# Attention in front of two feed-forward layers: the output product of a pair moved from step 3 to step 1, and its PV products spread over three steps instead of two

## The reference

```python
scores = q @ k.T / sqrt(64)                  # per batch (4) and head (8): 576 x 576
scores = where(block_i >= block_j, scores, -1e9)   # blocks of 64 rows and columns
attn = exp(scores - max(scores))
attn = attn / (sum(attn) + 1e-9)
x = attn @ v                                 # (4, 8, 576, 64) -> (2304, 512)
x = (sigmoid(x @ w_gate) * (x @ w_val)) @ w_out      # d_ff 1536
out = top-1 mixture of 8 experts (x, w_gate, w1, w2) # 2304 x 512
```

## Time and profile before

| | |
|---|---|
| median of 3 runs | 1006.93 us |
| lowest, highest | 1004.75, 1008.24 us |
| profiled execution, its own time | 1004.57 us |
| its span in the profile | 1002.8 us |
| PE busy over the span | 914.2 us (91%) |
| DVE, ACT, POOL busy | 338.6, 298.5, 253.0 us |
| attention | from 0 to about 230.7 us of the span |
| stretch 100 to 200 us: PE, DVE, ACT busy | 78.39, 65.16, 47.87 us of 100 |
| PE on the chain that ended last | 70% of the span |

### The profile page before, as it was taken

One profiled execution on the slowest core, in us unless ns is written; L12 is line 12 of the kernel. 1 busy time (PEld: TensorE's weight loads), 2 busy tenths in 40 slices (PEclk: granted clock), 3 DMA queues, 4 the chain that ended last, 5 costly groups with the idle time before them and its releaser, 6 DMA issues.

```text
span 1002.8 us, 15746 instructions
## 1 busy us (share of the span) xinstructions
PE 914.2 (91%) x5370; PEld 758.2 (76%) x5371; DVE 338.6 (34%) x635; ACT 298.5 (30%) x654; POOL 253.0 (25%) x249
## 2 busy tenths in 40 slices
PE   7788777769999999999999999999388998999995
PEld 3444444438999999999999999999367887888884
DVE  5665666662121110120120120111744445235421
ACT  4443444542222122112111211211254344125310
POOL 4033333311121111111111111111253445225521
PEclk9999999999999999999999999999689999999998
DMA  4443444432220010010010000000374547115310
GB/s 130 136 150 107 137 140 147 134 117 89 74 63 32 1 32 32 1 32 13 21 32 1 32 1 1 32 1 1 118 267 160 184 155 258 42 42 209 120 42 30
DMA packets 45536, 83.08 MB, mean 83 GB/s; under 512 B 6831, under 2 KB 19119, under 8 KB 45488
## 3 DMA queue, kind: packets, MB, share of 16 engines
q1 hardware_dynamic: 39728, 67.21, 20.8%
q0 software_dynamic: 3360, 10.49, 3.2%
q10 hardware_dynamic: 2400, 4.72, 1.2%
HBM read 68.17 MB, written 14.75 MB: 83 GB/s over the span
## 4 chain that ended last, share of the span: by engine, by line
PE 70%; POOL 2%; issue 2%; DMA 1%; DVE 1%; ACT 0%; POOLq 0%; ACTq 0%; SPq 0%; DVEq 0%
PE bank L1162 21%; PE bank L1163 21%; PE bank L1164 21%; PE bank L1299 2%; PE bank L1221 1%; DMA stage<-in_we 1%; POOL ew1l L368 1%; PE bank L1212 1%; PE bank L1273 1%; POOL ew2l L368 0%; PE bank L1129 0%; PE bank L1264 0%; POOL yg L598 0%; POOL out L615 0%; POOL ag L587 0%
## 5 line engine op out<-in xcount | busy, mean ns | idle before, releaser
L1162 PE MATMUL bank<-xh,w1h 128*128 128x384 f32 x576 | 196.1, 340 | 0.0
L1164 PE MATMUL bank<-xh,w1l 128*128 128x384 f32 x576 | 193.3, 336 | 0.0
L1163 PE MATMUL bank<-xl,w1h 128*128 128x384 f32 x576 | 193.2, 335 | 0.0
L573 POOL TENSOR_TENSOR hl<-hraw,hh 128x384 fp32r<-128x384 f32 x72 | 77.1, 1071 | 406.5 <-ACT hh L701 406.5
L889 DVE TENSOR_TENSOR hraw<-sig,bank 128x384 f32<-128x384 f32 x72 | 39.9, 554 | 349.2 <-ACT sig L730 349.2
L730 ACT ACTIVATE sig<-bank 128x384 f32<-128x384 f32 x72 | 35.4, 492 | 262.6 <-PE bank L1164 262.6
L672 ACT ACTIVATE prob<-bank,nmax 128x576 f32<-128x576 f32 (+2 forms) x144 | 76.1, 529 | 118.1 <-DVE nmax L842 112.9
L1162 PEld LDWEIGHTS bank<-xh,w1h 128*128 128x128 f32 x576 | 108.3, 188 | 1.8
L1163 PEld LDWEIGHTS bank<-xl,w1h 128*128 128x128 f32 x576 | 108.3, 188 | 1.7
L1164 PEld LDWEIGHTS bank<-xh,w1l 128*128 128x128 f32 x576 | 108.1, 188 | 0.0
L1090 PE MATMUL bank<-kt,qt 64*64 64x64 f32 (+7 forms) x640 | 71.7, 441 | 15.6 <-ACT prob L672 10.3
(11 more groups left out here) (147 smaller groups left out, 1306.8 us busy)
## 6 DMA issues: line engine op xcount, KB each, us to landing
stage<-in_we SPq DMA_DIRECT2D x56, 512.0 KB, 4.4
w1raw<-in_w SPq DMA_DIRECT2D x8, 768.0 KB, 5.5
kt<-in_kT SPq DMA_DIRECT2D x16, 288.0 KB, 3.7
qt<-in_qT SPq DMA_DIRECT2D x16, 288.0 KB, 4.2
rwide<-rinv_scratch SPq DMA_DIRECT2D x32, 144.0 KB, 3.1
xt_scratch<-xo SPq DMA_DIRECT2D x16, 288.0 KB, 2.1
xraw<-xt_scratch SPq DMA_DIRECT2D x6, 768.0 KB, 4.7
y_scratch<-yrow ACTq DMA_DIRECT2D x6, 768.0 KB, 3.6
```

Source lines behind the costliest of these rows:

```text
L573: pool.tensor_tensor(hl[:, f % 2, :], hraw[:, f % 2, :], hh[:, f % 2, :].bitcast(F32), ALU.subtract).then_inc(h_low, 1)
L1162: pe.matmul(out_, wh, ah, start=first, stop=False, skip_group_check=True)
L1163: pe.matmul(out_, wh, al, start=False, stop=False, skip_group_check=True)
L1164: return pe.matmul(out_, wl, ah, start=False, stop=last, skip_group_check=True)
```

## The change

It makes four edits:

1. The output product of pair g - 2 moves on DVE from step 3 to step 1.
2. PV's key tiles 3 and 4 move on PE from step 6 to step 8; tiles 1 and 2 stay in step 6, tile 0 in step 4.
3. SP stores `xo` before the reciprocals instead of after them, since the output product now comes ahead of the reciprocals.
4. After the last pair, DVE does the copy of unit 8, the output product of pair 14, the reciprocals of pair 15 and then the subtraction for `xl`.

```diff
-        PV_STEP = {4: [0], 6: [1, 2, 3, 4]}
-        RSUM_STEP, O_STEP = 2, 3
+        PV_STEP = {4: [0], 6: [1, 2], 8: [3, 4]}
+        RSUM_STEP, O_STEP = 2, 1
...
                 if not early:
-                    rinv_store(g - 2, p % 2)
                     if p == 3:
                         o_store(b, 0)
                     elif not isinstance(b, int):
                         o_store(b - 1, p + 1)
+                    rinv_store(g - 2, p % 2)
                     rwide_load(g - 2, p % 2)
...
             xload(0, PPB)
+            o_store(BATCH - 1, PPB - 3)
             rinv_store(NPAIR - 2, 0)
-            o_store(BATCH - 1, PPB - 3)
             rwide_load(NPAIR - 2, 0)
+            o_store(BATCH - 1, PPB - 2)
             rinv_store(NPAIR - 1, 1)
-            o_store(BATCH - 1, PPB - 2)
             rwide_load(NPAIR - 1, 1)
...
-            recips(NPAIR - 1, 1)
...
-            for i in range(NB - LAG, NB):
-                after_unit(NPAIR - 1, 1, i)
+            after_unit(NPAIR - 1, 1, NB - LAG)
+            after_unit(NPAIR - 1, 1, NB - LAG + 1)
+            o_out(NPAIR - 2, 0)
+            recips(NPAIR - 1, 1)
+            after_unit(NPAIR - 1, 1, NB - 1)
             xlow(0, 0)
-            o_out(NPAIR - 2, 0)
             o_out(NPAIR - 1, 1)
```

## The result

| | before | changed |
|---|---|---|
| median | 1006.99 us | 990.64 us |
| lowest to highest | 1004.75 to 1008.24 | 989.87 to 993.07 (4 runs) |
| profiled execution, its span | 1004.57, 1002.8 | 989.87, 988.2 |
| first feed-forward product | 230.74 | 213.01 |
| first w_out product | 243.33 | 226.23 |

The changed kernel is faster, by 16.4 us: ratio 0.9845, interval [0.9822, 0.9868]. The forecast was 982. The forecast for the first feed-forward product was a gain of 24.4; there the profiled execution is 17.7 ahead, and at its end 14.7.

What follows compares the result with a forecast made beforehand. No engine is full in attention; PE waits each pair for DVE's output product. Gains 14.6 (pairs) + 7.0 (end) + 2.8 (clock) - 0.2 = 24.2 us off 1004.57 give 980.4, stated as 982; range 970 to 992.

Steps and rivals of the forecast that it cites:

- the circle: Pair loop over DVE, ACT and PE: 13.50 us period, PE waiting for the output product before PV; 12.4 us forecast.
- half the gain: Rival for the whole kernel: splitting PV gives nothing and clock falls stay, gain 14.6 us, time 990; chance 0.18.
- The clock: PV steps behind two of fourteen waits for xo: both clock falls vanish with shorter waits, 2.8 us gained.
- The end of attention: Last pair to first feed-forward product: earlier transposes, product and PV at full clock gain 7.0 us; 5.5 without the clock.
- The output product to step 1: DVE, each pair: product ahead of the third reduction lets PV start 1.12 us earlier; 0.77 without earlier scores 1 and 2.
- PV in three steps: PE, each pair: moving key tiles 3 and 4 ends PE's 0.37 us idle and DVE's 0.35, total PE work unchanged.
- With the gap gone I take full clock: Last PV on PE: without the 4.76 us idle it runs at full clock, 3.1 us instead of 4.57, 1.5 gained.
- I take back 0.2: First w_out products: last output product ends only 3.2 to 4.4 us earlier, so 0.2 us of the gain is lost.
- The cover: Slack that keeps new waits away: 3.3 us at w_out, 2.5 us at K's scaling; rwide's load 4.3 us early.
- `rwide` late: Rival in step 1: the load of rwide lands too late and holds DVE and PE every pair, 1037 us; chance 0.05.

Runs made afterwards that it cites:

- e1: Changed kernel with PV back in two steps, so only the output product, SP's order and the end are changed: 994.07 us, ratio 0.9885.
- e2: Kernel before with PV in three steps and nothing else: 1005.49 us, ratio 0.9987.
- e7: Changed kernel as it is, timed and profiled a second time: 989.98 us, ratio 0.9823.
- e10: Changed kernel with the slice of w1 issued right behind the little store of the reciprocals instead of 4.4 us ahead: 989.17 us, ratio 0.9834.
- e3: Kernel before with only the new order after the last pair, on DVE and SP: 1002.68 us, ratio 0.9962.
- e4: Changed kernel with SP's old order, the little store of the reciprocals ahead of the big store of xo: 990.52 us, ratio 0.9832.
- e5: Changed kernel with the output product moved earlier again, to step 8 of the pair before: 991.15 us, ratio 0.9839.
- e6: e5 with PV in two steps, tiles 1 to 4 in step 6: 979.07 us, ratio 0.9726.
- e8: e6 with SP's old order, the little store of the reciprocals ahead of the big store of xo: 976.62 us, ratio 0.9696.
- e9: e6 with the slice of w1 issued right behind the little store instead of 4.9 us ahead of it: 977.05 us, ratio 0.9718.

## Why the prediction was right or wrong

The direction, the circle and the range were right; the time, 990.64 against 982, came out near the range's upper end, outside the 976 to 987 that the forecast's own sum had: the range held since it took in the rivals. That is the figure of the rival "half the gain", but only half for its reason: the clock falls stay, while the split does give something. Up to the PV step at 200.94 (212.84 before) 11.9 us were won, where the forecast says 13 x 1.12 + 1.12 + 2.8 = 18.5; from there to the first feed-forward product 5.8, where it says 24.4 - 18.5 = 5.9. Of the missing 6.7 the steps account for 6.5:

| step of the forecast | forecast | measured | missing |
|---|---|---|---|
| first reduction to PV | 4.65 | 4.73 | 14 x 0.08 = 1.1 |
| PV to the next first reduction | 7.73 | 7.87 | 13 x 0.14 = 1.8 |
| "The clock" | 2.8 | 0 (two falls before, two after) | 2.8 |
| intervals into pairs 4, 8 and 12 | as others | 12.76, 12.94, 12.86 | 0.7 |
| "The end of attention", from that PV step on | 5.9 | 5.8 | 0.1 |

The two intervals ahead of the loop are 12.46, together 0.3 us shorter than reckoned, and each fall costs 1.5 instead of 1.4, so the last digit of the sum means little.

- **"The output product to step 1": right in mechanism, too large.** e1 measured 0.61 for the part that the forecast put at 0.77. Three hand-offs make up the rest. The third reduction came 3.08 us behind the first (reckoned 3.05). From a third reduction to its exponential it is 128.66 - 127.93 = 0.73, and again 0.73 in e1; the forecast built 0.67 from duration and gap instead of reading it. The small transpose to PV is 123.69 - 123.35 = 0.34, reckoned 0.25. Together 0.03 + 0.06 + 0.09 = 0.18.
- **"PV in three steps ... PE's total is unchanged": this failed.** Scores 1 and 2 do start without a wait, and the start of the chain gains 5.17 - 4.73 = 0.44 over e1. But from PV to the next first reduction it is 7.87 (e2: 125.25 - 117.37 = 7.88) instead of 7.72 (e1) or 7.73, without a wait of PE that the profile shows. That 0.15 comes with cutting PV's second step in two; what in PE takes it isn't shown. Net 0.27 to 0.28 (e1 against the changed kernel, e2 against before), not 0.35.
- **"The clock. ... I count both falls as gone": this failed,** and was named as the least sure. The longest wait in a pair went from 1.8 to 1.08 us, and PV steps at half clock were still there: two in the changed kernel's profile, one in e7's, two in e10's. Before had two, e1 one, e2 four, e3 and e4 two, e5 three. Profiles without any in the pairs are those of e6, e8 and e9, where PE idles 0.2 to 0.4 at a time in most pairs. That the short waits are the cause isn't shown; these kernels differ in more than that.
- **"The end of attention": the sum was right, its clock by luck.** PV at full clock (3.08) is what this profile shows, but in e7, the same kernel, it took 4.40, and in e1, e3 and e4 5.77, 5.80 and 4.76. "With the gap gone I take full clock" holds in some executions only; e7 without it gives 17.90 - 13.93 = 4.0 from the PV step of pair 14 on, with the forecast's 1.12 of the pairs 5.1, near its 5.5.
- **"I take back 0.2" at w_out** measured 13.22 - 12.59 = 0.6. The last pair's little store, issued at 210.63, let the load go only at 214.32, 3.7 later: it ends at 214.1, 0.1 behind the big store issued at 209.88, which took 4.1, here with the last slice 14.8 us ahead. The last output product so ends at 217.80 + 1.32 = 219.1, 13.8 earlier than before, of which 11.9 are the pairs': 1.9, where the forecast had 3.2 to 4.4. The landings of the earlier trace rows had been read as if the new order left them alone. e4, with the old order, shows no such loss (12.61).
- **The cover held.** No product of the changed kernel waits for `rwide` inside the pairs and no scores wait for K, so the gain at feed-forward stayed but for those 0.6 and a part behind it. From the first router result to the end of the span it is 988.2 - 323.8 = 664.4 us, against 1002.8 - 340.8 = 662.0 before:

```profile
L878 DVE COPY logits<-bank x18: 159/167/169, 323.8 to 689.4; 128x8 f32<-128x8 f32 x18
```

  In the ten runs of the experiments that stretch is 662.0 to 666.4 long, 664.4 in e7 too. So the 2.4 lie within what it varies by from execution to execution, and the one shown of before was short there; the medians differ by 16.4, not 14.7. The forecast had noted the median 2.4 above the profiled execution and put it down to clock falls.
- **The rival "`rwide` late"** was right as a mechanism and wrong in place: it decides in e5, where the product comes a step sooner.

What decides in which pairs the clock falls stays open. The 0.7 us at the loop's round starts can be placed. In the steps of pair 8, DVE and ACT of the changed kernel, then DVE of the kernel before:

```profile
104.01 0.43 DVE L316 COPY pt<-bank 128x256 f32<-128x256 f32 x1 [1.52 <-PE bank L1103]
104.58 1.36 DVE L842 TENSOR_REDUCE nmax<-bank 128x1 f32<-128x576 f32 x2
```

```profile
105.46 0.74 ACT L672 ACTIVATE prob<-bank,nmax 128x576 f32<-128x576 f32 x1 [1.86 <-PE bank L1103]
```

```profile
112.75 1.57 DVE L842 TENSOR_REDUCE nmax<-bank 128x1 f32<-128x576 f32 x2
```

From DVE's last copy of a round to the first reduction of the next it is 104.58 - 104.01 = 0.57 us, within a round 131.40 - 131.05 = 0.35; from that reduction to its exponential it is 0.88, within a round 0.78. Together that is 0.32 of the 0.33 that the step into pair 8 costs. The kernel before has the same 0.57 and 0.88 there (copy at 112.18, exponential at 113.63). But it usually idles 0.35 ahead of the second reduction, and at 112.75 two reductions follow one another without that gap: the idle time takes the delay up. The split of PV removed this idle time and so laid the delay bare; e2 shows it too (0.08 to 0.32), e1, with PV in two steps, at most 0.13. What in the turn of the loop costs it isn't shown.

## What to carry to other kernels

An operation taken off the head of a wait is not free if it lands on another busy stretch of the same engine: look for a place where that engine itself waits (e6, 0.9 us per pair more than the change). Read hand-offs as distances between starts that stand in the trace, not as duration plus a guessed gap, since a circle repeated 13 times multiplies each 0.1. A small DMA that someone waits for should be issued ahead of the large ones, or so late that these have landed; and a gain that rests on the clock coming back should be left out of the sum and kept for the range.

## What the hardware showed that was not expected

- A store of 4.5 KB took 1.4 us in one pair and 4.1 in the next, by what was issued on the same queue up to 4.5 us ahead of it; with the same order and that transfer 6.0 us ahead it took 1.4 to 2.7.
- Cutting a run of 24 PV products into 16 and 8 cost PE 0.15 us per pair.
- With an idle time of 0.92 or 0.93 ahead of it, the last PV ran at full clock in one execution (3.08 us) and at half clock in another kernel's (5.80).
- In the changed kernel the step into a round of the loop costs 0.15 to 0.33 us more than a pair within it; in the kernel before an idle time of 0.35 us on DVE takes this up.
